# Decayed attention with a dense head: the attention stage laid out in 128 full lanes, with blocked decay products and an on-chip restack

## The reference

```
mag = sqrt(a_re*a_re + a_im*a_im)
scale = minimum(mag, 0.999) / (mag + 1e-6)
a_re_n, a_im_n = a_re*scale, a_im*scale
for t in range(768):
    new_re = ar*S_re - ai*S_im              # ar, ai: a_re_n, a_im_n at t
    new_im = ar*S_im + ai*S_re
    S_re, S_im = new_re + k_t v_t^T, new_im
    y[t] = q_t @ S_re
logits = x @ phi                            # x: y of all heads, 3072 x 384
d, c = softmax(logits, axis 0), softmax(logits, axis 1)
slot_out[e] = relu((d.T @ x)[e] @ w1[e]) @ w2[e]
x = c @ slot_out
out = relu(x @ w_in)**2 @ w_out
```

## Time and profile before

| | |
|---|---|
| runs (us) | 915.42, 922.25, 979.38; median 922.25 |
| span of the profiled execution | 920.3 us, 12655 instructions |
| TensorE busy | 772.9 us (84%) |
| VectorE busy | 605.0 us (66%) |
| ScalarE busy | 344.2 us (37%) |
| GpSimd busy | 381.7 us (41%) |
| HBM traffic | 82 GB/s over the span |

### The profile page before, as it was taken

The page is one execution under the profiler, slowest core; times in us unless marked ns, Lnnn a source line. Parts: engine busy times, 40 slices in busy tenths (PEclk is TensorE's granted clock), DMA queues, the critical chain, the costliest instruction groups (busy, mean ns, idle before and its releaser), DMA issues.

```text
span 920.3 us, 12655 instructions
## 1 busy us (share of the span) xinstructions
PE 772.9 (84%) x4142; PEld 515.1 (56%) x4142; DVE 605.0 (66%) x1792; ACT 344.2 (37%) x666; POOL 381.7 (41%) x399
## 2 busy tenths in 40 slices
PE   0003698888789899987989998999998999999997
PEld 0001355565556576655657775233336888888886
DVE  7999999999999998979986883200023333333332
ACT  5611453224642225542112331011134555555553
POOL 4483445345354334373332320000054555555553
PEclk9999557778865855567668998999999999999999
DMA  5011002222113131101236919556000000000000
GB/s 219 0 69 68 24 32 68 81 71 88 41 41 109 41 132 41 49 10 41 72 133 234 351 51 341 223 206 268 6 0 1 1 35 35 0 35 36 1 35 35
DMA packets 21025, 76.55 MB, mean 83 GB/s; under 512 B 1888, under 2 KB 11232, under 8 KB 18656
## 3 DMA queue, kind: packets, MB, share of 16 engines
q1 hardware_dynamic: 17504, 71.03, 21.0%
q10 hardware_dynamic: 3456, 4.72, 1.4%
HBM read 66.31 MB, written 9.44 MB: 82 GB/s over the span
## 4 chain that ended last, share of the span: by engine, by line
PE 55%; DVE 18%; issue 3%; ACT 1%; POOL 0%; ACTq 0%; DVEq 0%; POOLq 0%
PE ps L1171 7%; PE ps L1173 7%; PE ps L1172 7%; PE ps L1089 5%; PE ps L1109 5%; PE ps L965 4%; PE ps L984 3%; PE ps L1016 3%; PE ps L1020 3%; DVE ss L702 3%; DVE ee L678 3%; DVE et L673 2%; PE ps L1155 2%; DVE et L674 2%; DVE qk L819 2%
## 5 line engine op out<-in xcount | busy, mean ns | idle before, releaser
L965 PE MATMUL ps<-ident 128*32 128x512 bf16 x299 | 117.3, 520 | 90.7 <-DVE ee L678 80.3
L576 POOL TENSOR_TENSOR qk<-wi,ee 128x256 f32<-128x256 f32 x96 | 92.6, 965 | 243.2 <-DVE wi L804 165.7
L618 POOL TENSOR_TENSOR hlo<-qs,hhi 128x512 fp32r<-128x512 f32 x96 | 124.0, 1293 | 100.6 <-DVE qs L948 99.6
L948 DVE TENSOR_TENSOR qs<-rs 128x512 f32<-128x512 f32 x96 | 67.2, 700 | 147.2 <-ACT rs L511 147.2
L392 ACT ACTIVATE kts<-ps 128x256 f32<-128x256 f32 x80 | 30.7, 383 | 256.9 <-PE ps L972 256.9
L1171 PE MATMUL ps<-hhi,who 128*128 128x512 f32 x288 | 112.8, 392 | 1.7 <-POOL hlo L618 1.7
L1173 PE MATMUL ps<-hhi,wlo 128*128 128x512 f32 x288 | 112.6, 391 | 0.0
L1172 PE MATMUL ps<-hlo,who 128*128 128x512 f32 x288 | 112.5, 391 | 0.0
L965 PEld LDWEIGHTS ps<-ident 128*32 128x32 bf16 x299 | 27.3, 113 | 129.2 <-issue 106.0
L984 PE MATMUL ps<-qk 64*128 64x128 f32 x768 | 91.6, 370 | 2.8 <-DVE qk L819 2.8
L511 ACT ACTIVATE rs<-ps 128x512 f32<-128x512 f32 x96 | 57.5, 599 | 92.3 <-PE ps L1155 92.2
(11 more groups left out here) (146 smaller groups left out, 1255.5 us busy)
## 6 DMA issues: line engine op xcount, KB each, us to landing
wt<-in_w SPq DMA_DIRECT2D x16, 1536.0 KB, 8.6
aa<-in_a_all SPq DMA_DIRECT2D x8, 1536.0 KB, 7.3
xyr<-in_xy SPq DMA_DIRECT2D x24, 512.0 KB, 3.3
vr<-in_v_all SPq DMA_DIRECT2D x24, 192.0 KB, 3.5
x_scratch<-xsb ACTq DMA_DIRECT2D x24, 192.0 KB, 1.9
xs<-x_scratch SPq DMA_DIRECT2D x4, 1152.0 KB, 7.3
out<-ost SPq DMA_DIRECT2D x6, 768.0 KB, 3.5
wins<-in_w_in SPq DMA_DIRECT2D x1, 3072.0 KB, 13.7
```

Of the source, the lines that this page charges most:

```text
L618: pool.tensor_tensor(hlo[:, i % NHS, :], qs[:, i % NQS, :], hhi[:, i % NHS, :].bitcast(F32), ALU.subtract).then_inc(lo_ready, 1)
L965: nc.tensor.matmul(ps[0:SL, bank, :], idb[:, 0:SL], idle, start=True, stop=True)
```

## The change

The decays of a batch are laid in all 128 lanes: 16 groups of channels times 8 heads, with three channels a group along the columns. A batch's tile has 3 x 768 columns. Magnitudes, excess, normalising and scaled magnitudes are done for whole thirds (768 columns) ahead of the products, on ScalarE and VectorE. The running products are built in four blocks of 16 steps at once (`product_step`, 15 steps of 288 columns), and three `block_step`s multiply each block by the end of the one before (576 columns). Inverses come from suffix products and one scaling of 2304 columns.

Keys and queries of a chunk are made for all heads (`weigh`, `key_query`) into `xout`, with lanes by channel group and head. Six DMAs from SBUF to SBUF (`stack`) restack them into `stk`: 96 lanes (real and imaginary channels), columns by head. `scores` is then one matmul per head. The state's turn from chunk to chunk is a 96x96 matrix per head that VectorE builds (`build_turn`, from factors restacked by `stack_turns`), and TensorE multiplies by it: `turn_keys` for the keys, `next_state` for the state. GpSimd only makes constants in this stage. `keep_busy` is no longer called here. The expert weights are loaded earlier: three in the pass of the last products, three after the first restack of the last pass, two behind its last.

```diff
+            def stack(n):
+                sp.wait_ge(kq_ready, 4 * (n + 1))
+                if n >= NST:
+                    sp.wait_ge(y_done, n - NST + 1)
+                for c in range(2):
+                    for t in range(DT):
+                        k = c * D + t
+                        sp.dma_start(stk[k:k + DT * (DL - 1) + 1:DT, n % NST], xout[:, n % NOUT, c, t])\
+                          .then_inc(stacked[n % NST], 16)
...
+            def stack_turns(b):
+                sp.wait_ge(chain, C_ALL * b + C_TURN)
...
+                for c in range(2):
...
+                        sp.dma_start(gst[k:k + DT * (DL - 1) + 1:DT, b % 2],
+                                     gd[:, c, t].rearrange("p c g -> p (c g)")).then_inc(g_stacked[b % 2], 16)
...
+                for c in range(NC):
+                    n = (p - 1) * NC + c
+                    if c == 0 and p < B - 1:
+                        for t in range(DT):
+                            load_raw(p + 1, t)
+                    if p:
+                        stack(n)
...
+                    if c == NC - 2 and p < B:
+                        stack_turns(p)
+                    if c == 2 and p == B - 1:
+                        sp.wait_ge(an_ready, DT * B)
+                        sp.wait_ge(m_ready, 2 * B)
+                        for k in range(3):
+                            load_w(k)
+                    if c == 0 and p == B:
+                        sp.wait_ge(chain, C_ALL * (B - 1) + C_SCAN)
+                        sp.wait_ge(kq_ready, 4 * NC * (B - 1))
+                        for k in range(3, 6):
+                            load_w(k)
...
+            def sign_planes(b, t):
+                act.wait_ge(an_ready, DT * b + t + 1)
...
+                nc.scalar.activation(n0, p0, ACT.Copy, scale=-1.0).then_inc(signed, 1)
+                nc.scalar.activation(n1, p1, ACT.Copy).then_inc(signed, 1)
+                act.wait_ge(signed, 3 * (DT * b + t) + 2)
+                nc.scalar.activation(p1, p1, ACT.Copy, scale=-1.0).then_inc(signed, 1)
...
+                for c in range(NC + 3 * (p == B)):
+                    n = (p - 1) * NC + c
+                    if c == 0 and p < B:
+                        for t in range(DT):
+                            sign_planes(p, t)
+                        norm_squares(p)
...
+                        copy_lg(n - 3)
+                    if p < B - 1:
+                        if c == 1:
+                            for t in range(DT):
...
+            def normalise(b, t):
+                dve.wait_ge(p_ready, DT * b + t + 1)
+                dve.scalar_tensor_tensor(out=grid(PL[b % 2] + t * PT, [PF, 2], [1, PT]),
+                                         in0=grid(V_ + t * PT, [0, 2], [1, PT]), scalar=1.0,
+                                         in1=grid(RAW + t * PT, [PF, 2], [1, PT]), op0=ALU.subtract, op1=ALU.mult,
+                                         reverse0=True).then_inc(an_ready, 1)
...
+            def init_products(b):
+                done, e = C_ALL * b, PL[b % 2]
+                dve.wait_ge(signed, 3 * DT * (b + 1))
+                dve.wait_ge(an_ready, DT * (b + 1))
...
+            def product_step(b, i):
...
+                dve.wait_ge(chain, done)
+                dve.tensor_tensor(t1, grid(spot(e, i), [0, 2], *dims), grid(spot(e, i - 1), [PF, 2], *dims),
+                                  ALU.mult).then_inc(chain, 1)
+                dve.tensor_tensor(t2, grid(spot(N_, i), [e + PF - N_, 2], *dims),
+                                  grid(spot(e + PF, i - 1), [-PF, 2], *dims), ALU.mult).then_inc(chain, 1)
+                dve.wait_ge(chain, done + 2)
+                dve.tensor_tensor(grid(spot(e, i), [PF, 2], *dims), t1, t2, ALU.add).then_inc(chain, 1)
...
+            def block_step(b, k):
...
+                dve.tensor_copy(pexp[:].rearrange("p c t x i -> p (c t) x i"),
+                                grid(spot(e, BL * k - 1), [PT, 2 * DT], [2, CF], [0, 2])).then_inc(chain, 1)
...
+                dve.wait_ge(chain, done + 1)
+                dve.tensor_tensor(w1_, er, pr, ALU.mult).then_inc(chain, 1)
+                dve.tensor_tensor(w2_, ei, pi, ALU.mult).then_inc(chain, 1)
+                dve.tensor_tensor(w3_, er, pi, ALU.mult).then_inc(chain, 1)
+                dve.tensor_tensor(ei, ei, pr, ALU.mult).then_inc(chain, 1)
+                dve.wait_ge(chain, done + 4)
+                dve.tensor_tensor(er, w1_, w2_, ALU.subtract).then_inc(chain, 1)
+                dve.wait_ge(chain, done + 5)
+                dve.tensor_tensor(ei, ei, w3_, ALU.add).then_inc(chain, 1)
...
+            def suffix_step(b, k):
...
+                if k == 0:
+                    dve.wait_ge(m_ready, 2 * (b + 1))
...
+                here = grid(spot(m, i), [step_cols, tb], [2, CF])
+                dve.tensor_tensor(here, here, grid(spot(m, i + 1), [step_cols, tb], [2, CF]),
+                                  ALU.mult).then_inc(chain, 1)
...
+            def inverses(b):
...
+                dve.tensor_tensor(mm, mm, fx, ALU.mult).then_inc(chain, 1)
...
+            def weigh(n, f):
...
+                dve.tensor_tensor(x.rearrange("p t (j i) -> p t j i", i=2), x.rearrange("p t (j i) -> p t j i", i=2), m,
+                                  ALU.mult).then_inc(weighed, 1)
...
+            def key_query(n, inverse, f):
+                b, c = divmod(n, NC)
+                if inverse:
+                    dve.wait_ge(weighed, 2 * n + f + 1)
+                elif f == 0 and n >= NOUT:
+                    k = n - NOUT
+                    dve.wait_ge(stacked[k % NST], 96 * (k // NST + 1))
...
+                dve.tensor_tensor(o, e, x, ALU.mult).then_inc(kq_ready, 1)
...
+            def build_turn(n):
...
+                dve.tensor_tensor(o, i, g, ALU.mult).then_inc(rot_ready, 1)
...
+            def apply_mask(n, half):
...
+                dve.tensor_tensor(asb[:, n % 2, HB * half:HB * (half + 1), :], a, mk, ALU.mult).then_inc(masked, 1)
...
             for p in range(B + 1):
-                if p < B:
-                    start_products(p)
-                for i in range(NI + 4 * (p == B)):
-                    n = (p - 1) * NI + i
-                    if p < B and i == (SW0 if p else 2):
...
-                    if 0 <= n < B * NI - 1:
-                        others += [(inverse_weight, n + 1, 0), (inverse_weight, n + 1, 1)]
-                    others += [(update_state, dve, m, part) for m, part in updates_in(n) if m // NC >= LB]
-                    if 2 <= n < B * NI + 2:
-                        others.append((apply_mask, n - 2))
...
+                if 1 <= p < B:
+                    for t in range(DT):
+                        normalise(p, t)
+                for c in range(NC + 1 * (p == B)):
+                    n = (p - 1) * NC + c
+                    lo, mid, hi = c / NC, (c + 0.5) / NC, (c + 1) / NC
+                    if 0 <= n < NT:
+                        weigh(n, 0)
+                        weigh(n, 1)
+                        key_query(n, 0, 0)
+                        key_query(n, 0, 1)
+                        key_query(n, 1, 0)
+                        key_query(n, 1, 1)
+                        if has_turn(n):
+                            build_turn(n)
                     if p < B:
...
+                        parts_in(p, lo, mid)
+                    if 1 <= n <= NT:
+                        apply_mask(n - 1, 0)
+                        apply_mask(n - 1, 1)
+                    if p < B - 1:
+                        if c == 2:
+                            for t in range(DT):
+                                norm2(p + 1, t)
+                        if c == NC - 1:
+                            for t in range(DT):
+                                excess(p + 1, t)
...
-                        inverse_weight(n + 1, 1)
+                        parts_in(p, mid, hi)
+                    if p < B - 1 and c == NC - 1:
+                        for t in range(DT):
+                            scaled_mag(p + 1, t)
...
+                pe.wait_ge(stacked[n % NST], 96 * (n // NST + 1))
+                for half in range(2):
+                    if n:
+                        pe.wait_ge(masked, 2 * (n - 1) + half + 1)
+                    for h in range(HB * half, HB * (half + 1)):
+                        x = stk[0:KR, n % NST, h]
+                        last = nc.tensor.matmul(ps[:, half, (h % HB) * CH:(h % HB + 1) * CH], x[:, 0:CH], x[:, CH:2 * CH],
+                                                start=True, stop=True)
+                    last.then_inc(a_done, 1)
+
+            def turn_keys(n):
...
+                    if k:
+                        pe.wait_ge(kt_copied, 2 * (k - 1) + half + 1)
+                    for h in range(HB * half, HB * (half + 1)):
+                        last = nc.tensor.matmul(ps[:, 2 + half, (h % HB) * KR:(h % HB + 1) * KR],
+                                                stk[0:KR, n % NST, h, 0:CH],
```

(44 more changed lines are left out.)

990 lines of the change are left out of this document (383 added, 607 removed).

## The result

The changed kernel takes 992.74 us (median; 992.04 to 996.06) against 921.84 us of the kernel before, a ratio of 1.079 (95% interval 1.073 to 1.085). The forecast was 813 us, with a range of 770 to 915 us. The change makes the kernel 8% slower.

A forecast was written before the change was run, and what follows sets the result against it. It took VectorE to bound the kernel before, and VectorE and TensorE nearly level after, with the clock deciding: 101 + 4 x 83.5 + 9 + 5 + 6 = 455 us of attention plus 358 gives 813 us, range 770 to 915.

The forecast's parts named there:

- The tail and VectorE: Code behind attention keeps its 358 us; VectorE falls from 118 to 85.4 us in a middle batch.
- The pairs: Key/query products on VectorE read pairs 96 bytes apart; taken at the plain rate, 0.47 us each, with nothing added.
- The start: Before attention's first scores: products begin at about 34.8 us, first scores at about 101 us, paid once.
- TensorE's prices: Full matmul pass 0.217 us at low clock, 0.116 at full; 96-column weights taken as 0.163 and 0.087.
- I carry 0.72 over: TensorE's mean clock in attention stays 0.72 without idle matmuls, so a batch takes 83.5 us.
- Rival (b): TensorE's clock stays low because the filling matmuls are gone: 115.5 us a batch, 931 us in all; chance 0.15.
- the products of chunk n+1 stand ahead of that mask on VectorE while TensorE works on chunk n for 10 us or more, which covers it: Each chunk's restack of 5 to 6 us is hidden behind TensorE's work; uncovered it would cost 144 us.
- 9 for batch turns: ScalarE work ahead of a new batch's first chunk costs about 4.5 us at each of two batch turns.
- 5 for weights: A restack behind weight loads on SP stalls the scores of chunk 19 by 0 to 15 us; 5 taken.
- 6 for the end: Attention's end, with last outputs, copies, transposes and logits, takes 6 us.
- The sum: Attention takes 101 + 4 x 83.5 + 9 + 5 + 6 = 455 us; with 358 behind it, 813 us.
- Rival (c): The restack binds: its six moves run one after another, 21 us a chunk at 3.5 each, 973 us; chance 0.08.

The follow-up runs named there:

- e5: Changed kernel with values loaded one chunk later, expert weights behind the last restack and next batch's decays behind a pass's first restack, no filling: 931.80 us.
- e4: The kernel before, without its idle matmuls in attention: 952.54 us against 919.51 us.
- e6: e5 with twelve idle matmuls ahead of each chunk's scores: 873.92 us.
- e11: e9 with eight instead of twelve idle matmuls ahead of each chunk's scores: 808.14 us.
- e1: Changed kernel with SyncE's values load behind each restack asking for a chunk one earlier: 936.62 us.
- e9: e6 with turned keys and outputs alternating head by head and next state behind transposes and logits: 822.63 us.
- e12: e11 with SyncE's queue as in the changed kernel: 926.57 us.
- e7: e6 with eight more idle matmuls a chunk, one after each second head in outputs and next state: 925.94 us.

## Why the prediction was wrong

- **The tail and VectorE: right.** What follows attention took 359.3 us (forecast 358). Products began at 34.34 (forecast 34.8). A product step takes 1.36 us (forecast 1.32). Products and the preparation of the next batch take 52.1 us, from 34.34 to 86.42, where the next normalise starts (forecast 53.5). The pairs cost something after all: four key/query products take 2.15 from the first to the next operation, 0.54 each, between the plain 0.47 and the strided 0.70; 1.7 us a batch. The Trainium skill's rule that two hits on a line are enough for full rate ("SBUF — State Buffer", "Door 1: The DMA port swizzle") is nearly but not quite borne out. The lines of these:

```profile
34.34 0.46 DVE L577 TENSOR_TENSOR tt<-big 128x288 f32<-128x288 f32 x1
...
35.70 0.46 DVE L577 TENSOR_TENSOR tt<-big 128x288 f32<-128x288 f32 x1
...
92.04 2.23 DVE L700 TENSOR_TENSOR xout<-big,xq 128x384 f32<-128x384 f32 x4
94.19 0.95 DVE L713 TENSOR_TENSOR rot<-bm,gst 96x768 f32<-96x768 f32 x1
```

- **The start: nearly right.** First scores at 105.3 instead of 101. The first restack is issued from 94.3 to 98.1 (the sum has 95.7), but lands behind the next batch's decays, 2.3 MB issued at 88 on the same queue; in e5, where they stand behind it, the first scores start at 100.7.

- **TensorE's prices: right at either level.** 0.213 and 0.111 a pass against 0.217 and 0.116; 96-column weights 0.160 and 0.085 against the estimated 0.163 and 0.087. The count was a little off: a transpose is one record and not two (72 of L1030 in the kernel before, 72 of L954 after), so a batch has 406 full passes and not 424, 111.6 us instead of 115.5 at the low clock and 80.6 instead of 83.5 in the sum. And the 26.9 of VectorE has six turns in it, not five; five make 26.0.

- **The step that failed first: "I carry 0.72 over".** The term was 334 us (4 x 83.5). TensorE was busy for 428.75 from 105 to 630, 95 us more. The granted clock of a kernel with idle matmuls in it was carried to one without. I weighed the densest part of the new row for it, and the taking out of the filling against it, and had no row for either. e4 shows the price on the kernel before, e5 on the changed one, and e6 to e11 that filling and order bring it back. Rival (b) named this, with 0.15; it should have been the forecast. The Trainium skill, "TensorE: Matmul & The Clock Gate", "What's actually happening", says that a busy array gets its full clock; 90.00 busy us of 90 at 0.50 in e5 contradict it for these matmuls, as 330 to 370 of the earlier trace rows did.

- **The step that failed second: "the products of chunk n+1 stand ahead of that mask on VectorE while TensorE works on chunk n for 10 us or more, which covers it".** True of VectorE, which made them 11 us ahead; but I did not walk SyncE's own list. There the load of values for three chunks on stands ahead of the restack, and it waits for outputs. The order excerpt of SyncE in the section on the change has that row; I read the weights in it and passed over the values. The terms were 9 for batch turns, 5 for weights and 6 for the end, 20 in all. Restack waits were 93.7: about 38 in short ones behind the values load, 30 behind weights, 26 at the two batch turns. e1 took 56 us away with that one row.

- **The sum by these.** 105.3 + 428.8 + 93.7 + 2.7 of other idle time = 630.5, and 359.3 behind it make 989.8. Against 455 that is 4 + 95 + 76. Rival (b) alone gave 931; e5, which has the low clock and the batch turns left, measures 931.80. That the two agree so closely is partly luck: TensorE is busy there for 431.4 us and not 462, and waits for 31.2 us and not 10. Rival (c) put a price on a restack that is slow by itself; no run showed that.

- **The batch turns** were mis-sized: 4.5 us each in the sum, 10 to 17 in the changed kernel, e1, e5 and e11. A batch's last chunk has no turn and no next state, so TensorE is through early while VectorE still has scaled magnitudes, normalise, the next chunk's keys and queries and the first products ahead of the mask (179.8 to 194.0 in e11).

## What to carry to other kernels

A granted clock belongs to the row of matmuls that it was read from. When a change takes filling out or alters what TensorE does in a row, price TensorE at both levels and take the low one until a trace shows otherwise. For a transfer that is to be hidden, walk its queue's list row by row and ask of each row ahead what it waits for; "issued early enough" holds only if nothing ahead of it waits longer. And try such things together: here filling or the queue alone brought back 6%, both 12%, and both with a better order 19%; that order was worth 51 us with the queue mended and about 5 with the old one.

## What the runs showed of the hardware

- The clock of TensorE followed what stood side by side, not whether it was busy: 90 us at 1.2 GHz without a gap in e5, a fall amid the 48-column outputs in e6 without a gap either, and a mean of 0.88 in e9 by the same matmuls in another order. Which property of the matmuls counts (the columns that they move, their type, their weight loads) no run separates. Idle time also brings it down: in e12, with 57 us more of waits for the restack, the mean fell from 0.87 to 0.72. The Trainium skill, "TensorE: Matmul & The Clock Gate", "HAM oscillation — how this bites in real kernels", says this of waits, and e12 agrees; that it falls without a wait is what e6 adds.
- A clock row of 1.00 can stand for "nothing recorded". In the changed kernel up to 439 and in all attention of e1 the passes of 0.213 us show 1.2 GHz, and in that of e4 passes as long as in the earlier trace rows.
- A bf16 matmul among fp32 ones cost 0.42 us at full clock instead of 0.21 (e7); the weight load behind it did not start under it.
- Landing of a restack's 6 x 128 KB depended on what stood ahead: 16.80 us after the last issue behind 4.7 MB of weights, about 3.1 without (chunk 10: issued until 308.34, scores from 311.48).
